# Attention in pairs of heads: the softmax division moved behind the value product, and the operands of the scores assembled by transfers

## The reference, cut to what matters

```python
def _attn_ref(q, k, v, centroids):          # q, k, v: 2 x 8 heads x 768 x 64; 16 centroids of each head
    q_assign = argmax(q_n @ c_n.T)          # nearest centroid of each query row, k_assign likewise
    k_assign = argmax(k_n @ c_n.T)
    mask = q_assign[:, :, :, None] == k_assign[:, :, None, :]
    scores = scale * q @ k.T
    scores = where(mask, scores, -1e9)
    attn = exp(scores - max(scores))
    attn = attn / (sum(attn) + 1e-9)
    return attn @ v
...
x = attention output as 1536 tokens x 512
x = _moe_ref(x)      # x @ w_in (512 x 2048), a rational function of each element, @ w_out
x = _moe2_ref(x)     # 8 experts, each relu(x @ w1) @ w2, weighted by a Sinkhorn gate
```

## Time and profile before

| | |
|---|---|
| median of 3 runs | 1626.21 us (1625.97 to 1627.86) |
| the profiled execution's own time | 1633.07 us |
| its span | 1631.3 us |
| busy over the span | PE 96%, PEld 88%, DVE 68%, ACT 38%, POOL 39% |
| first and last exponential of attention | 21.7 and 335.0 us after the span's start |
| DMA | 67.93 MB, 13.9% of 16 engines |

### The profile page before, as it was taken

The page is one execution under the profiler, slowest core; times in us unless marked ns, Lnnn a source line. Parts: engine busy times, 40 slices in busy tenths (PEclk is TensorE's granted clock), DMA queues, the critical chain, the costliest instruction groups (busy, mean ns, idle before and its releaser), DMA issues.

```text
span 1631.3 us, 25695 instructions
## 1 busy us (share of the span) xinstructions
PE 1567.1 (96%) x8305; PEld 1434.4 (88%) x8305; DVE 1107.6 (68%) x2072; ACT 625.1 (38%) x1296; POOL 639.0 (39%) x484
## 2 busy tenths in 40 slices
PE   5888888889999999999999999999999999999998
PEld 5777777789999999889899899899998998998997
DVE  5888888889989885545565655655655655655655
ACT  5778888878777752012111111111111111111111
POOL 4667766620000022298424325325325325235220
PEclk9999999999999999999999999999999999999999
DMA  4222322120000010011011011011011011011002
GB/s 113 82 81 85 86 80 80 42 104 1 1 1 0 13 39 27 14 40 39 27 39 52 14 39 52 13 39 51 13 39 52 13 39 51 13 39 48 16 13 77
DMA packets 76196, 67.93 MB, mean 42 GB/s; under 512 B 17136, under 2 KB 58224, under 8 KB 76144
## 3 DMA queue, kind: packets, MB, share of 16 engines
q1 hardware_dynamic: 76144, 67.25, 13.9%
HBM read 64.09 MB, written 3.15 MB: 41 GB/s over the span
## 4 chain that ended last, share of the span: by engine, by line
PE 83%; DVE 8%; issue 5%; ACT 4%; DVEq 0%; POOL 0%; ACTq 0%; DMA 0%; POOLq 0%
PE ps L679 11%; PE ps L678 11%; PE ps L680 11%; PE ps L572 8%; PE ps L571 8%; PE ps L570 8%; PE ps L607 3%; PE ps L609 3%; PE ps L608 3%; PE ps L525 3%; PE ps L527 3%; PE ps L526 3%; DVE OH L981 2%; PE ps L501 1%; DVE PTl L1023 1%
## 5 line engine op out<-in xcount | busy, mean ns | idle before, releaser
L1204 DVE SCALAR_TENSOR_TENSOR acc<-ps,gate,acc 128x512 f32<-128x512 f32 x372 | 278.8, 749 | 186.5 <-PE ps L680 186.5
L678 PE MATMUL ps<-w2h,hh 128*128 128x512 f32 x768 | 299.1, 389 | 0.9 <-DVE acc L1201 0.9
L679 PE MATMUL ps<-w2l,hh 128*128 128x512 f32 x768 | 299.0, 389 | 0.0
L680 PE MATMUL ps<-w2h,hl 128*128 128x512 f32 x768 | 299.0, 389 | 0.0
L881 ACT ACTIVATE hh<-ps 128x384 fp32r<-128x384 f32 x256 | 119.6, 490 | 371.7 <-PE ps L572 211.2
L1167 DVE SCALAR_TENSOR_TENSOR hl<-ps,hh 128x384 fp32r<-128x384 f32 x256 | 141.3, 553 | 98.7 <-ACT hh L881 92.7
L919 ACT ACTIVATE p1s<-ps 128x384 f32<-128x384 f32 x56 | 27.5, 492 | 452.7 <-PE ps L572 452.7
L680 PEld LDWEIGHTS ps<-w2h,hl 128*128 128x128 f32 x768 | 144.2, 188 | 30.1
L678 PEld LDWEIGHTS ps<-w2h,hh 128*128 128x128 f32 x768 | 144.2, 188 | 29.5 <-DVE acc L1201 1.3
L679 PEld LDWEIGHTS ps<-w2l,hh 128*128 128x128 f32 x768 | 144.2, 188 | 28.0
L1351 POOL TENSOR_SCALAR w1h<-raw 128x1792 fp32r<-128x1792 f32 x28 | 47.8, 1708 | 285.6 <-PE ps L572 285.2
(11 more groups left out here) (155 smaller groups left out, 3612.1 us busy)
## 6 DMA issues: line engine op xcount, KB each, us to landing
raw<-in_w SPq DMA_DIRECT2D x64, 256.0 KB, 3.3
raw<-in_w SPq DMA_DIRECT2D x32, 512.0 KB, 3.4
qd<-in_qT SPq DMA_DIRECT2D x32, 192.0 KB, 3.2
kd<-in_kT SPq DMA_DIRECT2D x32, 192.0 KB, 3.1
wst_in<-in_w_in SPq DMA_DIRECT2D x16, 256.0 KB, 2.7
qk<-in_qT SPq DMA_DIRECT2D x16, 192.0 KB, 3.1
qk<-in_kT SPq DMA_DIRECT2D x16, 192.0 KB, 3.3
vraw<-in_v SPq DMA_DIRECT2D x16, 192.0 KB, 2.5
```

The lines of the kernel that those rows point to most:

```text
L678: pe.matmul(o, lh, w2h[b][:, fh, :], start=(fh == 0), stop=False)
L679: pe.matmul(o, lh, w2l[b][:, fh, :], start=False, stop=False)
L680: last = pe.matmul(o, ll, w2h[b][:, fh, :], start=False, stop=(fh == 1))
L1204: dve.scalar_tensor_tensor(out=acc[:, tt, :], in0=y, scalar=g, in1=acc[:, tt, :], op0=ALU.mult, op1=ALU.add).then_inc(y_added, 1)
```

## The change

What it does, by engine. A "pair" is two heads, 12 steps (s = 0 to 11; r is the head in the pair).
- **Division.** POOL no longer multiplies `Pb`. DVE takes the six reciprocals of a head at once (`reciprocals`, in the first step of the next head). SP writes them to DRAM as one row (`recip_to_row`, 768 elements of 4 bytes) and reads the row back to 64 partitions (`recip_to_rows`); POOL multiplies the value product by it (`x_scale`).
- **Value product.** ACT copies all 128 rows to `pvs`; two transfers (`pv_copy`) put its halves on the right partitions of `xsum` and `xlow`; POOL adds them, multiplies, and splits (`x_scale`, `x_lo`), ACT makes the high part (`x_hi`). DVE's addition is gone.
- **Operands.** q and k of two heads are loaded once, on 128 partitions. ACT makes `KH` and `QH` for the pair, POOL `KL` and `QL`. Six transfers for each head (`rows_copy`) and two for the mask (`mask_copy`) then put the halves on the rows of `K1`, `K2`, `Q1` and `Q2`.
- **Clusters.** One pass for a pair: `assign` works on 384 logits a partition, its multiplication by `desc` is POOL's (`rank`), the one-hot rows are one instruction of 384 elements, and ACT writes both halves of a transpose in one (`MR`).
- POOL makes the high parts of v and `w_in`, which were ACT's.

```diff
-            def load_win(n):
...
+            def rows_copy(m, r):
+
+                tiles, split = ((m - 1) * 2 + r + 1) * QT, m + 1
+                at_least(sp, scores_done, tiles)
+                carry_wait()
+                sp.wait_ge(q_lo, split)
+                src = slice(r * D, (r + 1) * D)
+                for dst, half, tile in ((K1, 1, KH), (K1, 0, KL), (K2, 0, KH), (Q1, 0, QH), (Q1, 1, QH), (Q2, 0, QL)):
+                    sp.dma_start(dst[half * D:(half + 1) * D, r, :], tile[src, :].bitcast(F32)).then_inc(rows_in[r], 16)
+            def mask_copy(m, r):
+                sp.wait_ge(mask_rows, (m + 1) * 2)
+                for dst, row in ((Q2, r * 32), (K2, D + r * 32)):
+                    sp.dma_start(dst[D:D + NC, r, :].rearrange("p (h s) -> p h s", h=2),
+                                 MR[row:row + NC, :, 0:HS]).then_inc(rows_in[r], 16)
...
+            def recip_to_row(n, r):
+                sp.wait_ge(sum_recip, n + 1)
+                sp.dma_start(row_d[r:r + 1, :].rearrange("a (t p) -> p (a t)", p=P), rrc(r * QT, QT),
+                             allow_slow_non_contiguous=True).then_inc(recip_out, 16)
...
             def scores(n, b, t, pair_of):
                 if t == 0:
-                    pe.wait_ge(mask_rows, (n + 1) * 2)
-                    pe.wait_ge(q_lo, n + 1)
-                    pe.wait_ge(k_lo, n + 1)
-                    pe.wait_ge(k2_hi, n + 1)
+                    pe.wait_ge(rows_in[b], pair_of * ROWS + ROWS)
...
-                    pe.wait_ge(norm_done, g1 + 1)
+                    pe.wait_ge(exp_done, g1 + 1)
...
+                if nxt and s in (0, 1):
+                    logits(pair + 1, s)
+                if nxt and s in (4, 6):
+                    onehot_transposes(pair + 1, (s - 4) // 2)
...
+                if nxt and s == 3:
+                    keys_hi(pair + 1)
+                if nxt and s == 4:
+                    queries_hi(pair + 1)
+                if nxt and s in (5, 7):
+                    mask_to_rows(pair + 1, (s - 5) // 2)
+                if s == 8 and current and not (isinstance(pair, int) and pair == 0):
+                    x_hi(pair - 1)
...
+                    act.activation(pvs[:], ps[:, 6, 0:HS], ACT.Copy).then_inc(pv_copied, 1)
...
+                if t == 0 and not first:
+                    reciprocals(n - 1, 1 - r)
+                if nxt and s == 2:
+                    assign(pair + 1, 0)
...
+                if nxt and s == 3:
+                    assign(pair + 1, 1)
...
+                if s in (3, 8):
+                    win_piece(pair * 2 + s // 8, s // 8, pair)
+                if nxt and s == 2:
+                    rank(pair + 1)
+                if nxt and s == 4:
+                    keys_lo(pair + 1)
+                if s == 4:
+                    values(pair * 2 + 1, 1, pair)
+                if nxt and s == 5:
+                    queries_lo(pair + 1)
+                if s == 7 and started:
+                    x_scale(pair - 1)
+                if s == 9 and started:
+                    x_lo(pair - 1)
+                if nxt and s == 10:
+                    values((pair + 1) * 2, 0, pair + 1)
```

More of the change, by code:

```diff
@@ L49 @@
 OHW = 112
+NP = BH // 2
 def at_least(eng, sem, value):
@@ L334, in _ @@
             sp.dma_start(ident[:], ident_d).then_inc(ident_in, 16)
[L336 to L351, removed]
@@ L760, in emit, with x_hi @@
+            def x_hi(m):
+                act.wait_ge(x_scaled, m + 1)
+                hi, raw = (x[:].rearrange("p a k s -> p (a k s)")[:, bass.ds(m * S, S)] for x in (XTh, xsum))
+                act.activation(hi, raw, ACT.Copy).then_inc(xt_hi, 1)
+            def emit(pair, s, current, nxt):
+                r, t = divmod(s, QT)
+                n = pair * 2 + r
                 g = n * QT + t
@@ L783, in emit @@
                                        ACT.Copy).then_inc(pt_hi, 1)
-                if t == (4 if current else 5) and b == 0 and not first:
-                    act.wait_ge(x_done, n * 2)
-                    flat = XTh[:].rearrange("p a k s -> p (a k s)")
-                    act.activation(flat[:, bass.ds((pair - 1) * S, S)], xt[:], ACT.Copy).then_inc(xt_hi, 1)
                 if t in (0, 3) and not first:
@@ L847, in mlp_step @@
                     wout_piece_hi(f)
+                if first and f == 4:
+                    x_hi(NP - 1)
                 if f == 3 and not first:
@@ L1094, in x2_lo_part @@
                                       ALU.subtract).then_inc(x2_lo, 1)
-            for p in range(5):
+            for p in range(2):
                 assign(0, p)
@@ new lines, in x_lo, with emit @@
+            def x_lo(m):
+                pool.wait_ge(xt_hi, m + 1)
+                carry_wait()
+                hi, raw, lo = (x[:].rearrange("p a k s -> p (a k s)")[:, bass.ds(m * S, S)] for x in (XTh, xsum, XTl))
+                lo_part(lo, raw, hi).then_inc(xt_lo, 1)
+            def emit(pair, s, current, nxt):
+                r, t = divmod(s, QT)
+                if not current:
+                    return
+                started = not (isinstance(pair, int) and pair == 0)
+                if s in (3, 8):
[14 more added lines that the diff above has]
+                    values((pair + 1) * 2, 0, pair + 1)
@@ L1305, in _ @@
+            keys_lo(0)
+            queries_lo(0)
+            rank(0)
+            values(0, 0, 0)
             steps(emit)(pool)
+            x_scale(NP - 1)
+            x_lo(NP - 1)
             def add(dst, x, y):
```

506 lines of the change are left out of this document (258 added, 248 removed).

## The result

The changed kernel takes 1669.4 us (median of 4 runs, 1668.26 to 1674.77) where the kernel before took 1626.35 beside it: 1.0269 times as long, interval 1.0246 to 1.0292. The forecast was 1561.9 and its range ended at 1604; the side was wrong too. The profiled execution has a span of 1666.0 us.

A forecast was written before the change was run, and what follows sets the result against it. No single engine bounds attention; the chain of steps through DVE sets the beat. Savings 52.2 (six middle pairs) + 4.7 + 6.9 - 1.0 + 1.5 = 64.3 us, from 1626.2 to 1561.9; range 1542 to 1604.

The forecast's parts named there:

- The new wait: Before a head's scores in attention: eight transfers must land first; predicted 2.0 us early, so nothing waits.
- My other end: Operand transfers before scores: 4-byte pieces cost several times one of v's and copies run at half rate, +6 us.
- both of its rivals: Late operands before scores: 1590 us, chance 0.27; or late past break-even: 1643 us, chance 0.05.
- 2.0 us of slack: Before scores in attention: operand rows land at 17.6 us, PE needs them at 19.6.
- rival *slower: Operands before scores come past the 10.7 us break-even, a pair 11.6 us longer: 1643 us, chance 0.05.
- what would prove me wrong: Profile signs in attention: PE waiting for operand transfers, ACT waiting at pvs, KH or x_hi, or PE long at half rate.
- the rival's evidence: For operands late before scores (1590 us, chance 0.27): 33 transfers a pair instead of 16, SP standing still for reciprocals.
- The sum: Whole kernel, savings in attention and behind it less prologue cost: 64.3 us saved.
- The operands' cover: Before scores in attention: operand rows arrive 2.0 us early, so PE does not wait for them.
- The OH instruction: DVE's one-hot rows, once a pair in attention: 0.55 us, or about 2.3 if held.
- The prologue: Before the first exponential: six transfers and rank join its chain, but the mask's chain ends last; costs 1.0 us.
- +1.5 behind the last exponential: Between attention and MLP: POOL's multiplication and a copy to XTh leave the way, saving 1.5 us.

The follow-up runs named there:

- row_apart: Changed kernel with the reciprocals' 768 pieces of 4 bytes written 64 bytes apart in DRAM, rb read from v: 1587.44 us, ratio 0.9743.
- no_recip: Changed kernel with reciprocals neither written to DRAM nor read back, POOL multiplying by ones: 1571.11 us, ratio 0.965.
- no_recip_small: no_recip with each operand copy cut to an eighth of its bytes from the third pair on: 1571.27 us, ratio 0.9639.
- write_only: no_recip plus the write of the reciprocals as 768 neighbouring 4-byte pieces, which nothing waits for or reads: 1642.47 us, ratio 1.0067.
- row_512b_early: Changed kernel with reciprocals transposed by PE, written as six 512-byte pieces, row and read back earlier in SP's order than in row_512b: 1579.41 us, ratio 0.9687.
- late_read: Changed kernel with the row written as before but its read back issued later in SP's order: 1661.29 us, ratio 1.0194.
- row_512b: Changed kernel with reciprocals transposed by PE, written as six 512-byte pieces, write and read later in SP's order: 1634.71 us, ratio 1.0033.

## Why the prediction was wrong

**The step that failed** is in "The new wait": "and v, 768 pieces of 256 bytes, lands in 2.5. I take those values." The same number of pieces was taken for the same time. Measured, the 768 pieces of 4 bytes take 10.3 us (median of 16) from issue to release of SP, 4.1 times as long, and it is their lying side by side that does it (with their order, see row_apart): 4.0 when 64 bytes apart. My other end, "every piece of 4 bytes costs several times one of v's", was near it: +6 for the row and slow copies together, where the row alone is 7.8 over 2.5. I put it aside for a load of as many pieces, when the rows of the trace have no write to DRAM at all. A price with no near row should have got more chance than the 0.32 that both of its rivals had together.

**The place was wrong as well.** I looked for the late row at the scores, with 2.0 us of slack. From 60 to 340 us no wait for scores names it. What waited was the buffer that I had left out: `pvs` is a single one, its two transfers stand directly behind the row in SP's order, and ACT, whose queue holds the exponentials, can't copy the next half before both are through. My rival *slower* (1643, chance 0.05) had the row at 5 instead of 2.5, but took it through the operands, which needed 10.7 us of delay to break even; by way of `pvs` there was next to no slack (even in no_recip ACT waits there, 5.8 us in six waits). I had written "ACT waiting at `pvs`" under what would prove me wrong, without ever counting it. The transfers behind `pvs` are not forced either: the kernel before has ACT move the half (`vpart`, L794) from partitions 64 to 127 to partitions 0 to 63 in the same 0.49 us. (So ACT need not write on the partitions that it reads.) The Trainium skill's port rule, "SBUF — State Buffer", section "Door 1: The DMA port swizzle", gave 1.3 us more for the copies; by no_recip_small the copies' bytes cost nothing as long as the row is away, so no run here shows it to matter. The rule that mattered was the one on completions, cited under write_only, and the prediction did not weigh it.

**SP standing still** was counted as nothing ("SP stands still for the return of the reciprocals" stands under the rival's evidence alone). With the slow row SP's standing, the read back and POOL's wait for it add 2.0% together (1.0269 against 1.0067), some 33 us; with a quick one 0.2%.

**What held**, by no_recip, which is the change without that row:
- The sum. 1633.07 - 1569.56 = 63.5 between the profiled executions, forecast 64.3 with the row counted as free.
- A pair: 31.14, forecast 31.4; last exponential 269.9 (273). The single steps did not come as forecast: 2.05 to 2.1 was expected in steps 10, 11 and 1, and the pair above has 1.62, 2.03 and 1.62 there, the short ones right behind steps with a late `pvs` copy.
- DVE's wait for the exponential, 0.2 us a step before, is gone: no wait of DVE names an exponential any more.
- The operands' cover: in no_recip no wait of PE for `K1`, `K2`, `Q1` or `Q2` is among the waits of 60 to 270 us.
- The OH instruction: forecast 0.55, or 2.3 if held by `KL`; it takes 1.73 in the middle pairs, one for two heads, beside `KL`.

**Smaller errors.** They partly cancel, so that the sum came out within 1 us is in part luck. DVE's addition of 1e-9 to six sums was counted with the four small instructions of 0.6 in all; in no_recip each takes 0.91, two a pair. The six copies were to be issued in 3.3 to 3.5; they take 4.3 and 4.8 in the pair above, so about 1 of the 2.0 of slack went there. The prologue was to cost 1.0; the first exponential comes 3.1 later. In the working itself, 8.9 and six times 0.55 make 12.2 and not 12.4, and two sets of logits 2.8 and not 2.7. +1.5 behind the last exponential did not come: 1567.6 - 269.9 = 1297.7 against 1296.3. The 4.7 of the first pair and 6.9 of the last were not separated. And the base: the profiled execution of before was 6.9 over its median, that of no_recip 1.5 under its own, so the same 63.5 are 55 to 57 us in medians; taking the whole sum off the median made the forecast some 8 us too low even for the kernel without the row.

**What stays open.** The stage runs at a clock of 0.85 and not 0.98 as in row_512b_early. In the changed kernel PE is busy for 0.24 us between 142 and 146, while ACT waits for `pvs` (until 145.25), and its granted clock is 0.50 from 146 to 152. So part of the 98 us is PE at half rate after its waits. POOL's waits for `win_raw` (133.1, 52.5 without the row) stand ahead of `KL` and `QL` in its order and may delay them. Neither share was measured by itself; both fall when the row goes. Order and place of the pieces were not separated either.

## What to carry to other kernels

A transfer is priced by its pieces' size and place as well as by their number, and a few KB written element by element can be the dearest on the chip: shape it first (here a transpose by PE to six pieces of 512 bytes), or bound it by a separate run before a sum rests on it. Ask of each slow transfer not only who waits for it but what is issued behind it, and which single buffers those transfers empty. And when a wait is moved in a queue written by hand, look for the one that takes its place: in late_read and row_512b ACT waits 44 and 55 us behind a read back that came too late.

## What the runs showed that was not expected

- 768 pieces of 4 bytes side by side in DRAM, 3 KB in all, take 10.3 us (median) to complete; 64 bytes apart, and in another order, 4.0; as 128 pieces of 24 bytes, 3.3.
- Transfers issued behind such a write completed together with it, with the DMA engines at 0.00 for 4 us (write_only), and transfers of SP land late even when ACT's queue issued the write (7.4 against 4.0).
- The write is slower under load: 8.4 us (median) at a DMA share of 0.38, 10.3 at 0.56, and the copies' bytes, free without it, cost 38 us with it.
